# Query decays multiplied from their bank, weighted values and output gating moved from VectorE to GpSimd

## What is computed

```python
for t in range(S):
    m_new = np.maximum(f_gate[:, :, t] + m, i_gate[:, :, t])
    f_stab = np.exp(f_gate[:, :, t] + m - m_new)
    i_stab = np.exp(i_gate[:, :, t] - m_new)
    C = f_stab * C + i_stab * einsum('bhd,bhe->bhde', vt, kt)
    n = f_stab * n + i_stab * kt
    denom = maximum(abs(n . q), 1.0)
    y[:, :, t] = sigmoid(o_gate) * (C . q) / denom
```

## Time and profile before

| | |
|---|---|
| time, median of 3 runs | 692.22 us (691.65 to 697.82) |
| span of the profiled execution | 693.2 us (no separate time is recorded for it) |
| TensorE busy | 668.9 us, 96% |
| VectorE busy | 264.9 us, 38% |
| GpSimd busy | 186.7 us, 27% |
| ScalarE busy | 175.2 us, 25% |

### The profile page before, as it was taken

The page is one execution under the profiler, slowest core; times in us unless marked ns, Lnnn a source line. Parts: engine busy times, 40 slices in busy tenths (PEclk is TensorE's granted clock), DMA queues, the critical chain, the costliest instruction groups (busy, mean ns, idle before and its releaser), DMA issues.

```text
span 693.2 us, 9936 instructions
## 1 busy us (share of the span) xinstructions
PE 668.9 (96%) x3702; PEld 538.6 (78%) x3702; DVE 264.9 (38%) x446; ACT 175.2 (25%) x342; POOL 186.7 (27%) x151
## 2 busy tenths in 40 slices
PE   3998979999999999999999999999999999999998
PEld 1787768777777777777788888888888888888887
DVE  9769999523352223222323213132221322313122
ACT  5234434322242224222321112111111211211211
POOL 6825697000880000000680004810038200000000
PEclk9569997999999999999999999999999999999999
DMA  8144552000130000000130000310002000001011
GB/s 269 57 123 138 173 158 89 1 1 0 46 107 15 1 0 0 0 0 0 46 107 15 0 0 30 107 30 0 0 28 89 19 0 0 0 0 38 0 38 38
DMA packets 19283, 30.59 MB, mean 44 GB/s; under 512 B 3296, under 2 KB 12128, under 8 KB 19264
## 3 DMA queue, kind: packets, MB, share of 16 engines
q1 hardware_dynamic: 19264, 30.33, 14.4%
HBM read 28.36 MB, written 1.97 MB: 44 GB/s over the span
## 4 chain that ended last, share of the span: by engine, by line
PE 86%; DVE 10%; issue 2%; ACT 1%; DVEq 1%; ACTq 0%
PE bank L483 40%; PE bank L585 9%; PE bank L587 8%; PE bank L586 8%; PE bank L490 5%; PE bank L531 4%; PE bank L537 4%; PE bank L534 2%; PE bank L366 2%; DVE qd L789 2%; PE bank L386 1%; PE bank L394 1%; DVE pr L778 1%; DVE mem L794 1%; DVE vw L784 1%
## 5 line engine op out<-in xcount | busy, mean ns | idle before, releaser
L483 PE MATMUL bank<-xx,wab 128*128 (+1 forms) x840 | 219.3, 400 | 0.2 <-DVE xx L803 0.2
L483 PEld LDWEIGHTS bank<-xx,wab 128*128 128x128 f32 x840 | 152.5, 188 | 41.0 <-issue 10.2
L903 DVE SCALAR_TENSOR_TENSOR act_l<-bank,act_h 128x512 fp32r<-128x512 f32 x96 | 66.3, 692 | 248.9 <-ACT act_h L712 248.9
L712 ACT ACTIVATE act_h<-bank 128x512 fp32r<-128x512 f32 x96 | 57.5, 599 | 285.7 <-PE bank L490 164.5
L305 POOL TENSOR_TENSOR wab<-raw,zeros 128x768 fp32r<-128x768 f32 (+2 forms) x32 | 41.6, 1299 | 214.3 <-PE bank L537 125.2
L483 PE MATMUL bank<-xx,ex 128*128 x336 | 85.8, 394 | 0.0
L483 PEld LDWEIGHTS bank<-xx,ex 128*128 128x128 f32 x336 | 60.9, 188 | 12.1 <-issue 1.5
L864 DVE TENSOR_TENSOR prod<-prod,bank 128x512 f32<-128x512 f32 x36 | 24.8, 689 | 114.5 <-PE bank L483 114.5
L585 PE MATMUL bank<-ex,act_h 128*128 128x320 f32 x192 | 61.3, 319 | 1.2 <-DVE act_l L903 1.2
L585 PE MATMUL bank<-wab,act_h 128*128 128x320 f32 x192 | 61.3, 319 | 0.0
L586 PE MATMUL bank<-wab,act_h 128*128 128x320 f32 x192 | 59.3, 309 | 0.0
(11 more groups left out here) (122 smaller groups left out, 874.1 us busy)
## 6 DMA issues: line engine op xcount, KB each, us to landing
raw<-w SPq DMA_DIRECT2D x16, 320.0 KB, 2.9
raw<-w SPq DMA_DIRECT2D x16, 256.0 KB, 2.6
nat_s<-nat SPq DMA_DIRECT2D x12, 324.0 KB, 4.4
qk_s<-qk SPq DMA_DIRECT2D x24, 160.0 KB
raw<-w SPq DMA_DIRECT2D x16, 128.0 KB, 2.7
tok<-o_gate SPq DMA_DIRECT2D x3, 640.0 KB, 5.5
raw<-w_out SPq DMA_DIRECT2D x6, 320.0 KB, 3.3
raw<-w_a SPq DMA_DIRECT2D x4, 384.0 KB, 8.0
```

What stands on the lines that cost most here:

```text
L483: last = nc.tensor.matmul(psum, a, b, start=start and i == 0, stop=stop and i == len(passes) - 1)
L712: nc.scalar.activation(act_h[:, f % 2, :], bank[f % 4][:, :], ACT.Relu).then_inc(hh_ready, 1)
L903: nc.vector.scalar_tensor_tensor(act_l[:, f % 2, :], bank[f % 4][:, :], 0.0, act_h[:, f % 2, :].bitcast(F32), ALU.max, ALU.subtract).then_ ...
```

## The change

1. **Query decays.** ScalarE writes the exp of `ps_q` back into `ps_q` and no longer into `eg`. VectorE's `qd` reads queries from SBUF and decays from the bank. The last column of each pair, which the update of the memory needs, is first written by a small exp of its own (128x4) into `eg_last`. TensorE may overwrite `ps_q` only when `qd` has been made, so `query_exponents(n+1)` now waits for `qd_ready` and stands behind `carried_outputs(n)`.
2. **Weighted values.** `vw` is made by GpSimd (`weigh_values`), two instructions a step, which wait for the decays of that step.
3. **Output gating.** The two gating instructions are made by GpSimd (`gate_outputs`), once the quotient is there (new semaphore `quo_ready`). TensorE's `turn_outputs(n)` waits for the quotient of step n-1, where it waited for its gating. The wait ahead of tile 4 stays one for the gating of step 11.
4. **Order on GpSimd.** Its loop over the MLP pieces becomes a loop over steps: weigh the values of step n+1, gate the outputs of step n-1, then as many pieces as SyncE loads for step n (none, one from n = 2, two from n = 8). The rest follow after the last gating.

The diff, cut to its core:

```diff
+            def mlp_piece(i):
                 pool.wait_ge(raw_in[i % 2], mlp_at[i])
-                split_piece(kind, i % 2, i, None, None)
+                split_piece(mlp_pieces[i], i % 2, i, None, None)
+                pool.wait_ge(pieces_split, i + 1)
+
+            def weigh_values(n):
...
+                if n >= 2:
+                    pool.wait_ge(upd_ready, n - 1)
+                for g in range(2):
+                    heads = slice(g, H, 2)
+                    pool.wait_ge(decay_ready, 2 * n + (g + 1))
+                    v = nat_s[:, s, DM:DM + H * V1].rearrange("p (h v) -> p h v", h=H)[:, heads, :]
+                    nc.gpsimd.tensor_tensor(vw[:, b, heads, :], v, dec[:, b, g, :, P - 1:P].to_broadcast([P, PAIRS, V1]), ALU.mult).then_inc(vw_ready, 1)
+
+            def gate_outputs(n):
+
+                b, at = n % 2, ((n % 2) * NC + n // 2) * XW
+                pool.wait_ge(quo_ready, n + 2)
+                nc.gpsimd.tensor_tensor(tok[:, at + DM:at + XW], quo[:, b, 2 * P:DM], tok[:, at + 2 * P:at + DM], ALU.mult).then_inc(rest_gated, 1)
+                pool.wait_ge(rest_gated, n + 1)
+                nc.gpsimd.tensor_tensor(tok[:, at:at + DM], quo[:, b, :], tok[:, at:at + DM], ALU.mult).then_inc(x_ready, 1)
+
+            pool.wait_ge(ogate_ready, NBLK)
+            weigh_values(0)
+            piece = 0
+            for n in range(STEPS):
+                if n + 1 < STEPS - 2:
+                    weigh_values(n + 1)
+                if n > 0:
+                    gate_outputs(n - 1)
+                for _ in range(0 if n < 2 else 1 if n < 8 else 2):
+                    mlp_piece(piece)
+                    piece += 1
+            gate_outputs(STEPS - 1)
+            for i in range(piece, NMLP):
+                mlp_piece(i)
...
                 if not first:
-                    pe.wait_ge(eg_ready, n)
+                    pe.wait_ge(qd_ready, n)
...
+                    carried_outputs(n, b)
                     if nxt:
                         query_exponents(n + 1, ahead[1], 1 - b)
-                    carried_outputs(n, b)
...
-                nc.scalar.activation(eg[:, b].rearrange("p a t -> p (a t)"), ps_q[:, :], ACT.Exp).then_inc(eg_ready, 1)
+                by_pair = ps_q[:, :].rearrange("p (a t) -> p a t", a=PAIRS)
+                nc.scalar.activation(eg_last[:, b], by_pair[:, :, P - 1:P], ACT.Exp).then_inc(last_ready, 1)
+                act.wait_ge(last_ready, n + 1)
+                nc.scalar.activation(ps_q[:, :], ps_q[:, :], ACT.Exp).then_inc(eg_ready, 1)
...
-                nc.vector.tensor_tensor(qd[:, b], qk_s[:, s, 0], eg[:, b], ALU.mult).then_inc(qd_ready, 1)
+                nc.vector.tensor_tensor(qd[:, b], qk_s[:, s, 0], ps_q[:, :].rearrange("p (a t) -> p a t", a=PAIRS), ALU.mult).then_inc(qd_ready, 1)
```

More of the change, by code:

```diff
@@ L74, in _build @@
         pr = sb("pr", [P, 2, 2, PAIRS, P], F32, attn)
[L75 removed]
+        eg_last = sb("eg_last", [P, 2, PAIRS, 1], F32, attn)
         qd = sb("qd", [P, 2, PAIRS, P], F32, attn)
@@ L334, in split_piece @@
                                                   (low[0:REST, :, 1], raw_low[0:REST, :, 1], low[0:REST, :, 1])], number)
-            for i, kind in enumerate(mlp_pieces):
+            def mlp_piece(i):
                 pool.wait_ge(raw_in[i % 2], mlp_at[i])
-                split_piece(kind, i % 2, i, None, None)
+                split_piece(mlp_pieces[i], i % 2, i, None, None)
+                pool.wait_ge(pieces_split, i + 1)
+            def weigh_values(n):
+                s, b = n % 4, n % 2
+                if n < 4:
+                    pool.wait_ge(nat_in[s], 16)
+                else:
+                    pool.wait_ge(nat_in[s], 16 * (n // 4 + 1))
+                if n >= 2:
[25 more added lines that the diff above has]
+                mlp_piece(i)
             pool.wait_ge(block_done, 1)
@@ L387, in carried_outputs, with own_outputs @@
                                      skip_group_check=True)
-            def own_outputs(n, s, b):
+            def own_outputs(n, use, s, b):
+                pe.wait_ge(nat_in[s], 16 * (use + 1))
                 pe.wait_ge(probs_ready, 2 * n + 2)
@@ L409, in turn_outputs @@
                 pe.wait_ge(ot_copied, n + 2)
-                pe.wait_ge(x_ready, n + 1)
+                pe.wait_ge(quo_ready, n + 1)
                 for p in range(PAIRS):
@@ L429, in steps @@
                         turn_x(3)
-                    own_outputs(n, s, b)
+                    own_outputs(n, cc, s, b)
                     if more or s < 2:
@@ L444, in turn_x @@
                     pe.wait_ge(mem_ready, STEPS)
+                    pe.wait_ge(x_ready, 2 * TPB + 1)
                 elif i == 1:
-                    pe.wait_ge(eg_ready, STEPS)
+                    pe.wait_ge(qd_ready, STEPS)
                 else:
@@ L521, in down @@
                 if j == 0 and first:
-                    pe.wait_ge(x_ready, STEPS + 1)
+                    pe.wait_ge(x_ready, STEPS + 2)
                     pe.wait_ge(xl_ready, TPB)
@@ L772, in _, with probabilities @@
             other_parts(1, g_t)
-            def probabilities(n, use, s, b, g, update=True):
-                heads = slice(g, H, 2)
-                dve.wait_ge(nat_in[s], 16 * (use + 1))
+            def probabilities(n, use, s, b, g):
                 dve.wait_ge(decay_ready, 2 * n + (g + 1))
@@ L779, in probabilities @@
                                         ALU.mult).then_inc(probs_ready, 1)
[L781 to L784, removed]
             def decayed_queries(n, use, s, b):
@@ L793, in update_memory @@
                 for p in range(PAIRS):
-                    last = nc.vector.scalar_tensor_tensor(mem[:, b, p, :], mem[:, b, p, :], eg[:, b, p, P - 1:P], ps_u[:, p * P:(p + 1) * P],
+                    last = nc.vector.scalar_tensor_tensor(mem[:, b, p, :], mem[:, b, p, :], eg_last[:, b, p, :], ps_u[:, p * P:(p + 1) * P],
                                                           ALU.mult, ALU.add)
@@ L832, in steps @@
                         decayed_queries(n + 1, *after[1:])
-                        probabilities(*after, 0, update=more or s < 1)
+                        probabilities(*after, 0)
                     if more or s < 2:
@@ L836, in steps @@
                     if nxt:
-                        probabilities(*after, 1, update=more or s < 1)
+                        probabilities(*after, 1)
                     if more or s < 2:
```

21 lines of the change are left out of this document (8 added, 13 removed).

## The result

The changed kernel takes 720.83 us (median of 4 runs, 718.20 to 727.57), 1.0415 times the kernel before (95% interval 1.0358 to 1.0472). It is slower by 4.2%; 715 was forecast, and 703 to 725 was the range.

A forecast was written before the change was run, and what follows sets the result against it. VectorE was taken to bound the attention steps before, SyncE's queue behind GpSimd's pieces after. 692.2 us plus 14.5 (later last stage), 2.1 (wait at tile 4) and 6.0 (clock) gave 714.8, say 715; range 703 to 725.

The forecast's parts named there:

- SyncE's order as the price: Attention: queries queue behind piece loads waiting for GpSimd's splits, which wait for decays; last stage starts 14.5 us later.
- The gain that was to be hidden: Attention steps: with VectorE relieved, 6.5 us each instead of 8.04, 12.3 us over eight steps if nothing else held.
- Rival 2: Attention: VectorE stops being the bound and SyncE never holds TensorE up; 12.3 us back, 680 us; chance 0.05.
- The terms of the body: GpSimd's step: vw 0.5, gatings 1.3, piece 3.4 us; done 9.4 us after S(m), TensorE's start of step m's own outputs.
- The landing: Query loads behind weights: 3.8 us from split to landing, 4.3 behind two transfers; then 1.7 us from scores to own outputs.
- The start: Step 2's own outputs on TensorE: start at 51.2 us in either kernel, set by TensorE's half clock.
- The clock: TensorE falls to half clock after waits: 3.0 us at step 8, 1.5 at step 9, 1.5 for smaller waits; 6.0 together.
- Rival 1: Same chain of waits, but TensorE's clock stays high or recovers at once; 709 us; chance 0.27.
- the chain without a clock term: Attention: step starts from bodies, landings and 6.5 us steps alone; last stage at 137.4 us, a shift of +14.5.
- Rival 4: Attention: pieces, vw or landings at their upper bounds with every clock fall in full; 725 to 729 us; chance 0.09.
- Rival 5: VectorE stays slow despite the change; its time equals the forecast's, so it has no chance of its own.
- rival 3: Last stage: queries in time, but GpSimd's backlog holds tile 4 for 9.4 us; net -2.9, 689 us; chance 0.07.

The follow-up runs named there:

- experiment 1: Changed kernel with only SyncE's order edited: each piece load issued behind the queries of step m+4 instead of m+2; 682.56 us, ratio 0.9820.
- experiment 3: Kernel before with one edit on GpSimd: each weight piece waits for the next step's decays, no work moved; 715.76 us, ratio 1.0310.
- experiment 6: Kernel before, with weight pieces waiting for the next step's decays and SyncE issuing piece loads behind later queries; 681.02 us, ratio 0.9851.
- experiment 4: Kernel before run once more unchanged, for a second profile; one execution, 696.37 us.
- experiment 5: Kernel before with only GpSimd's first weight piece waiting for the first decays of step 1; 695.70 us, ratio 1.0037.
- decays_only: Kernel before with only the query-decay part of the change; vw and gating stay on VectorE, pieces split as they land; 682.02 us, ratio 0.9845.
- gate_first: Changed kernel with one edit on GpSimd: pieces 12 and 13 split behind the last gating instead of ahead; 715.75 us, ratio 1.0308.

## Why the prediction was right, and where its terms were off

- **The direction and the cause hold.** The forecast named SyncE's order as the price, waits for the query DMA ahead of the scores in steps 7 and 8 (those of steps 8 and 9), no wait for vw, SyncE waiting for splits. All stand in the profile, and experiments 1, 3 and 6 tie them to the queue: the wait put in alone brings 3.1%, the order on SyncE takes it away in both kernels.
- **The gain that was to be hidden is there.** 6.5 us a step was the estimate, and 6.18 was measured in experiment 1; the 0.3 us lie around the two waits of the step it was read from; experiment 1 has no such waits. Rival 2 described a true effect. It needed the edit of experiment 1 to come out.
- **The terms of the body**: the small exp 0.2 (0.17), vw 0.5 (0.47), gating 1.3 (0.32 + 0.86 = 1.18), a piece 3.4 (94.24 to 97.57, 3.3), the wait at tile 4 2.1 (2.14). From S(7) = 88.33 to the split of piece 5 it took 9.24 us, 9.4 were worked out.
- **The landing was taken too short.** The prediction took 3.4 us, the least landing of nat, plus the piece's issue: 3.8 and 4.3. From the end of the releasing split to the first score it took 5.4 for S(8) (97.57 to 102.95) and 5.3 for S(9), and behind two transfers 6.5 for S(4) (51.81 to 58.31) and 6.3 for S(7) (80.45 to 86.71). All lie above the upper bound as well, 4.8 (5.3 behind two transfers). The least of a row was used for a load that goes out in a burst with 320 or 384 KB of weights ahead of it; its median, 4.4, would have been nearer. Four such landings lie on the path, which runs as in the prediction through S(4), S(5), S(7), S(8) and S(9): S(7)'s scores waited 0.34 us for their own queries, so S(6)'s landing didn't decide. Together they took 2.2 + 2.0 + 1.6 + 1.5, some 7.2 us more than worked out.
- **The start was taken as unchanged, which was wrong by 8.7 us the other way.** "From S(2) = 51.2, which TensorE's half clock sets in either kernel": S(2) was 42.54. With piece 0 no longer beside it, VectorE's first qd takes 0.69 us instead of 1.71, TensorE's wait of 0.36 us at 27 us is gone, and the clock rises at 28.5 instead of 46.4. Experiments 4 and 5 show that holding the pieces brings it, and decays_only speaks for the wait as what counts and not GpSimd's work: there piece 0 is split at 25 us as before, but qd reads a bank and takes 0.69 us, TensorE doesn't wait, and the granted clock of 31 to 34 us is 1.00 (0.50 before). It swaps two groups of TensorE's matmuls as well, so the wait is not alone in it.
- **The clock.** Rival 1 falls: the half clock followed both long waits for some 11 us, as the last four rows of the stage table show. At S(8) the term had its upper bound right: from S(8) to the vw that waits for the next decays it took 6.7 us (105.92 to 112.62) where a step at the full clock takes 4.3 (88.33 to 92.60), and through the scores ahead of S(9) 3.0 (125.71 to 128.68) for 1.7, so 2.4 + 1.3 = 3.7 us against a bound of 3.8, with 3.0 taken. What was too small is the 1.5 us for "all" smaller waits. Behind the 4.88 us ahead of S(4) the clock fell just as far: the scores took 3.0 us again, and the step from S(4) to S(5) 9.9 where 6.5 were worked out, together 4.7 us on the path. At S(9) 1.5 was taken and it was 3.1: the same 1.3 through the scores, and 10.3 us from S(9) to S(10) for 8.5. Behind tile 4 it cost 1.6 us.

In sum: the chain without a clock term had the last stage at 137.4, and it began at 146.32. Those 8.9 us are -8.7 from the start, +7.2 from the landings and +10.4 for the rest: the half clock (6.0 had been taken), less about 1 for bodies a little shorter than worked out. So a gain of 8.7 us and losses of 11.6 us, none of them in the forecast, cancelled but for 2.9. The mechanism was right, but that the time fell into the range was luck: with S(2) at the 51.2 that the prediction took, the same chain would have ended 8.7 us later, near 729.5 (an estimate from these rows), above the 725. A forecast of +22.6 us met +27.3 in span: 23.4 up to the last stage, 2.1 at tile 4, the rest behind it. Rival 4, which had a chance of 0.09, was true in two of its parts, the landings and the clock, and not in pieces, vw and gating. Rival 5 wasn't needed, and rival 3's sum came close in the kernel of experiment 1 (9.4 against 9.92).

The contention of VectorE's two-input instructions with GpSimd, which rival 2 took from the Trainium skill (SBUF — State Buffer, "Who interferes with whom"), agrees with all runs: with one operand in a bank qd stays at 0.68 to 0.69 us beside a busy GpSimd. The prediction left out the section's exception for instructions with one input: it counts copies and `tensor_scalar` among what can contend, under conditions on their operands. The 1.21 us of the 12-column `tensor_scalar` in experiment 6 agree; it ends at 115.29, as the GpSimd instruction beside it does (115.26).

## What to carry to other kernels

Before work moves onto an engine, list who waits for that engine's other work, and what stands behind those waits in their queues: here nothing waited for GpSimd's weight pieces during attention except the load of a later piece, and behind that load stood the queries. Giving work to an idle engine in program order also gives its old work all the waits of the new; keep urgent loads ahead of patient ones in the issuing queue by more steps than the new order delays. When a row's durations spread widely, take for a burst the value of the bursts, not the least.

## What the runs showed of the hardware that was not expected

- TensorE's clock at the start seems to hang on one short wait. In both profiles of the kernel before it worked from 28 to 46 us almost without a gap at a granted clock of 0.50; in every profile without its wait of 0.36 us at 27 us (the changed kernel and all experiments but the repeat of the kernel before) the clock had risen by 31 us. Why a wait of 0.36 us is followed by 18 us at the half clock is open. So is whether every execution of the kernel before does so: its quickest, 687.3 to 689.3 us, had a mean granted clock of 0.975 to 0.980 against 0.967 and 0.961 in the two profiles, and have no trace.
- The full clock comes back at different times behind the same wait: from 128 to 134 us the granted clock was 0.50 in the changed kernel and 0.74 in gate_first, which run the same instructions up to there. That is 3 us of difference without an edit.
- The values (`nat_s`), the last load of a burst of about 1 MB, took 4.6 to 5.0 us to land in the seven bursts of the changed kernel from 50 us on, where before the least was 3.4 and the median 4.4. How much of it is due to the weights ahead was not tried.
